# One sine of one column ahead of ScalarE's first work, in a retention, mixer and MLP kernel

## The chip, the cores and the metric

The kernel runs on one core of one Trainium2 chip. The metric is the device time of one execution in microseconds (us); of several executions the median counts.

## The reference

Three layers follow one another, in float32, for 2 batches of 768 tokens with 8 heads of 64 channels (512 channels):

```python
# retention: per head, decaying state
state = gamma * state + k_t (x) v_t ;  y_t = scale * q_t @ state
# mixer with phases
theta = x @ w_theta
zr, zi = x * cos(theta), x * sin(theta)
u = x + (w_tok_r over tokens of zr) + (w_tok_i over tokens of zi)
x = u + relu(u @ w_ch)
# token MLP, then channel MLP
u = x + (relu(x^T @ w_tok1) @ w_tok2)^T
out = u + relu(u @ w_ch1) @ w_ch2
```

ScalarE computes the cosines and sines; everything else that it does is copying, `Abs` and `Relu`.

## The kernel before, in words

Each engine has its own hand-written program (the functions under `block.sync`, `gpsimd`, `scalar`, `vector`, `tensor`), and semaphores order them against one another. A matmul of float32 quality is made of three in the `F32R` type: every operand is split into a high part (a copy in `F32R`) and a low part (the rest), and `three` (L619 to L624) multiplies high with high, high with low and low with high.

The first stage takes the tokens in 12 chunks `g` of 128 (6 for each batch). For a chunk:

- SyncE loads `qkv_in` (`load_chunk`, L241 to L246), three buffers; a weight piece (`load_piece`, L248 to L251, 512 KB, three buffers `stage`) goes between chunks. Both wait on the queue for the work that frees their buffer; piece `i` from the fourth on waits for the low part of piece `i - 3`.
- PE computes the scores (L639), VectorE multiplies them with the decay mask `causal` (`prob`, L473), PE forms the outputs (L669, L679) and the chunk's key-value product (L653). GpSimd multiplies keys with their decay (`k_dec`, L291) and the old state with its decay (`carried`, L300), and VectorE makes the new `state` (L483, L486). VectorE then writes the chunk's result into `res` (L492).
- ScalarE copies that result into `x_hi` (`x_high`, L359), VectorE makes `x_lo` (L497), and PE computes theta: 12 matmuls at L622 with the two pieces of `w_theta` in `w_sq`. Of each weight piece, ScalarE makes the high part (`piece_high`, L352) and VectorE the low part (`piece_low`, L466 or L468). The two pieces of `w_theta` are split in chunk 0, behind that chunk's `x_hi` and `x_lo`.
- theta is folded into half a turn (L367 on ScalarE, L506 and L509 on VectorE); `waves` (L370 to L377) takes `Abs`, a sine for the cosine (with a bias from the constants) and a sine; VectorE multiplies both with the transposed chunk (L515, L518).

In the order written out for VectorE, the mask of chunk `g + 1` (`weigh`) stands ahead of `x_low(g)`. PE's order is at L725 on: the scores of the next chunk come behind the outputs, and theta of a chunk one round later.

From 95 us on PE runs the token mixing, the channel product, the token MLP and the channel MLP, with high parts from ScalarE and low parts from VectorE or GpSimd.

The constants are one array `cst`: ScalarE issues the transfer of its first 277 columns as its first instruction (L388), and SyncE that of the rest. `idle` is a tile of zeros that VectorE writes first of all (L533); PE multiplies it with itself twice while the first chunk is under way. The build puts `ACT_TABLE_LOAD` instructions, which no line of the kernel asks for, into ScalarE's program, each with the line of the activation behind it. In the program before there are two: one ahead of the first copy, and one ahead of the first sine.

ScalarE's program around the change, up to the loop:

Of the kernel before, what the change touches and what calls it, by code (L numbers as in the profile page):

```python
# [7 lines left out]
ACT = mybir.ActivationFunctionType  # L8

P = 128  # L10
# [63 lines left out]
def retention_mixer_mlp(nc, qkv, weights, consts, out):  # L74
    with ExitStack() as ctx:
        def sb(name, shape, dt=F32, within=ctx):
            return within.enter_context(nc.sbuf_tensor(name, shape, dt))

        def sem(name):
            return ctx.enter_context(nc.semaphore(name))  # L80

        cst = sb("cst", [P, N_CONST])
        causal = sb("causal", [P, 2, 4 * P])
        stage = sb("stage", [P, NSTAGE, PIECE])

# [23 lines left out]
        with ExitStack() as warm:  # L109
            idle = sb("idle", [P, DM], within=warm)  # L110
# [72 lines left out]
        idle_ready = sem("idle_ready")  # L183
# [165 lines left out]
        def _(act):  # L349
# [36 lines left out]
                act.activation(u[:, b, 0, k, :], res[:, b, k, :], ACT.Copy).then_inc(ut_hi, 1)  # L386

            act.dma_start(cst[:, 0:C_OUT], consts[:, 0:C_OUT]).then_inc(const_in, 16)  # L388
            act.wait_ge(const_in, 16)
            for g in range(NG + 2):  # L390
                if g < NG:
# [520 lines left out]
```

## Time and profile before

| | |
|---|---|
| median of 3 runs | 461.89 us (461.87 to 463.2) |
| profiled execution, own time | 461.14 us |
| its span, first to last instruction | 459.1 us |
| busy: PE, DVE, POOL, ACT | 449.8, 160.1, 123.3, 104.4 us |

The profile is of one execution, and all times in it count from the start of its span; the 2.0 us between span and time lie outside it. Engines: PE is TensorE, DVE VectorE, ACT ScalarE, POOL GpSimd, SP SyncE. A name such as L622 is a line of the kernel before. "Idle before" is the time in which an engine had nothing to run ahead of an instruction, with the instruction or transfer that ended it.

### The profile page before, as it was taken

The page shows a single profiled execution, that of the slowest core. Times are in us where ns is not written, and L with a number is a line of the kernel's source. Part 1 is how long each engine was busy: PE and PEld are TensorE (multiplying, and loading weights), DVE is VectorE, ACT ScalarE, POOL GpSimd, SP SyncE. Part 2 cuts the span into 40 slices and gives each one's busy share as a digit, 9 for nine tenths or more (in the row PEclk, how much of TensorE's full clock was granted, in tenths as well). Part 3 has the DMA queues.
Part 4 walks back from the last instruction along what each step waited for, and adds up shares of the span by engine and source line. Part 5 has one row for each costly group of instructions (what it writes and reads, how often), then busy time and mean ns, then how long its engine had stood idle before and what let it go on. Part 6 is the DMA issues. An engine that isn't in the chain of part 4 may idle for free.

```text
span 459.1 us, 6208 instructions
## 1 busy us (share of the span) xinstructions
PE 449.8 (98%) x2748; PEld 394.5 (86%) x2748; DVE 160.1 (35%) x227; ACT 104.4 (23%) x157; POOL 123.3 (27%) x80
## 2 busy tenths in 40 slices
PE   7899999999999999999999999999999999999996
PEld 4677877999999999999989988888888888888885
DVE  3789999743211220225335411111311112111112
ACT  0365555632022120002123311111111111111110
POOL 1422320326063141499934880000000000000000
PEclk9999999999999999999999999999999999999999
DMA  8955570042000000044420000000200000200002
GB/s 307 415 216 206 226 275 1 0 129 101 1 0 1 1 0 1 1 140 165 156 91 1 0 1 0 0 1 0 93 0 0 1 0 15 78 0 1 0 0 93
DMA packets 8458, 31.21 MB, mean 68 GB/s; under 512 B 880, under 2 KB 2032, under 8 KB 7024
## 3 DMA queue, kind: packets, MB, share of 16 engines
q1 hardware_dynamic: 8288, 30.67, 18.1%
q8 instruction: 22, 0.36, 0.3%
q10 hardware_dynamic: 144, 0.14, 0.2%
q14 instruction: 4, 0.03, 0.0%
HBM read 27.67 MB, written 3.15 MB: 67 GB/s over the span
## 4 chain that ended last, share of the span: by engine, by line
PE 95%; DVE 2%; DMA 1%; ACT 1%; issue 0%; DVEq 0%; ACTq 0%
PE ps L622 85%; PE ps L679 2%; PE ps L639 2%; PE ps L693 2%; PE ps L776 1%; DMA cst<-consts 1%; PE ps L653 1%; PE ps L669 1%; DVE res L616 1%; DVE prob L473 1%; ACT L359 0%; DVE causal L535 0%; DVE w_sq L468 0%; ACT w_sq L352 0%; DVE z_split L523 0%
## 5 line engine op out<-in xcount | busy, mean ns | idle before, releaser
L622 PE MATMUL ps<-u,w_a 128*128 128x512 f32 x432 | 103.3, 390 | 0.0
L622 PEld LDWEIGHTS ps<-u,w_a 128*128 128x128 f32 x432 | 81.1, 188 | 16.7
L610 DVE SCALAR_TENSOR_TENSOR w_sq<-ps,w_sq 128x512 fp32r<-128x512 f32 x36 | 24.9, 692 | 156.7 <-ACT w_sq L447 156.7
L622 PE MATMUL ps<-w_a,z_split 128*128 128x384 f32 x384 | 68.5, 336 | 0.2 <-DVE z_split L523 0.2
L622 PEld LDWEIGHTS ps<-w_a,z_split 128*128 128x128 f32 x384 | 66.6, 188 | 0.6 <-issue 0.5
L447 ACT ACTIVATE w_sq<-ps 128x512 fp32r<-128x512 f32 x36 | 21.5, 599 | 168.1 <-PE ps L622 168.1
L622 PE MATMUL ps<-w_sq,z_split 128*128 128x512 f32 x216 | 51.9, 389 | 0.0
L622 PE MATMUL ps<-w_sq,w_b 128*128 128x512 f32 x216 | 51.4, 390 | 0.0
L622 PEld LDWEIGHTS ps<-w_sq,z_split 128*128 128x128 f32 x216 | 40.6, 188 | 8.4
L622 PEld LDWEIGHTS ps<-w_sq,w_b 128*128 128x128 f32 x216 | 40.6, 188 | 8.4
L622 PE MATMUL ps<-u,w_sq 128*128 128x384 f32 x192 | 35.1, 338 | 0.0
L622 PE MATMUL ps<-w_b,z_split 128*128 128x384 f32 x192 | 34.4, 335 | 0.0
L622 PEld LDWEIGHTS ps<-w_b,z_split 128*128 128x128 f32 x192 | 33.4, 188 | 0.0
L622 PEld LDWEIGHTS ps<-u,w_sq 128*128 128x128 f32 x192 | 33.2, 188 | 0.0
L622 PE MATMUL ps<-w_sq,x_hi 128*128 128x512 f32 x96 | 30.7, 401 | 1.8 <-DVE w_sq L468 1.8
L530 DVE TENSOR_TENSOR res<-ps,res 128x384 f32<-128x384 f32 x16 | 8.2, 553 | 64.6 <-PE ps L622 64.6
L306 POOL TENSOR_TENSOR z_split<-z,z_split 128x768 fp32r<-128x768 f32 x8 | 15.7, 1959 | 45.1 <-ACT z_split L381 45.1
L291 POOL TENSOR_TENSOR k_dec<-qkv_in,cst 128x512 f32<-128x512 f32 x10 | 13.7, 1373 | 38.8 <-DMA qkv_in<-qkv 38.8
L381 ACT ACTIVATE z_split<-z 128x768 fp32r<-128x768 f32 x16 | 12.6, 838 | 44.2 <-PE ps L622 44.2
L311 POOL TENSOR_TENSOR u<-res,u 128x768 fp32r<-128x768 f32 x8 | 15.4, 1936 | 24.2 <-ACT u L386 24.2
L622 PEld LDWEIGHTS ps<-w_sq,x_hi 128*128 128x128 f32 x96 | 17.2, 189 | 5.0 <-issue 2.0
L622 PE MATMUL ps<-w_sq,x_lo 128*128 128x512 f32 x48 | 18.8, 392 | 0.0
(67 smaller groups left out, 463.7 us busy)
## 6 DMA issues: line engine op xcount, KB each, us to landing
stage<-weights SPq DMA_DIRECT2D x28, 512.0 KB, 3.3
qkv_in<-qkv SPq DMA_DIRECT2D x11, 1024.0 KB, 5.8
cols_out<-res SPq DMA_DIRECT2D x12, 256.0 KB, 2.3
qkv_in<-qkv SPq DMA_DIRECT2D x2, 512.0 KB, 5.1
cst<-consts SPq DMA_DIRECT2D x1, 256.0 KB, 5.7
cst<-consts ACTq DMA_DIRECT2D x1, 138.5 KB, 4.8
```

Source lines behind the costliest of these rows:

```text
L291: pool.tensor_tensor(heads(k_dec[:, n % 2, :]), heads(qkv_in[:, g % NQ, 2 * DM:3 * DM]), key_decay, ALU.mult).then_inc(key_ready, 1)
L306: pool.tensor_tensor(z_split[:, n % 2, 1, 0, :], z_blk[:, n // NK, 0, n % NK, :], f32(z_split[:, n % 2, 0, 0, :]), ALU.subtract).then_inc( ...
L311: pool.tensor_tensor(u[:, b, 1, k, :], res[:, b, k, :], f32(u[:, b, 0, k, :]), ALU.subtract).then_inc(ut_lo, 1)
L381: act.activation(z_split[:, n % 2, 0, a, :], z_blk[:, n // NK, a, n % NK, :], ACT.Copy).then_inc(z_hi, 1)
L447: act.activation(h2[:, f % 2, 0, :], bank(BK_H2 + f % 4), ACT.Relu).then_inc(h2_hi, 1)
L473: dve.tensor_tensor(prob[:, :, :], ps[:, BK_SCORE:BK_SCORE + 2, :], causal[:, :, :], ALU.mult).then_inc(prob_ready, 1)
L530: dve.tensor_tensor(part, ps[:, BK_MIX + 2 * (n % 2) + half, 0:HS], part, ALU.add).then_inc(y_kept, 1)
L610: dve.scalar_tensor_tensor(out=h2[:, f % 2, 1, :], in0=bank(BK_H2 + f % 4), scalar=0.0, in1=f32(h2[:, f % 2, 0, :]), op0=ALU.max, op1=ALU. ...
L622: mm = pe.matmul(dst, left(l), right(r), start=first and n == 0, stop=last and n == 2, skip_group_check=True)
L639: mm = pe.matmul(ps[:, BK_SCORE + r, i * P:(i + 1) * P], qkv_in[rows, g % NQ, DM + i * P:DM + (i + 1) * P], qkv_in[rows, g % NQ, i * P:(i ...
L679: mm = pe.matmul(ps[cols, BK_Y + r, i // 2 * P:(i // 2 + 1) * P], qkv_in[:, g % NQ, 3 * DM + h * D:3 * DM + (h + 1) * D], prob[:, r, i * P ...
L693: mm = pe.transpose(ps[:, BK_XROW, k * P:(k + 1) * P], res[:, b, k, c * P:(c + 1) * P], ident)
```

## The change

ScalarE gets two instructions behind its first transfer: it waits for `idle`, and takes the sine of one column of it. The result goes to a new tile `spare` that nothing reads. `spare` stands behind `cst` in memory.

```diff
         cst = sb("cst", [P, N_CONST])
+        spare = sb("spare", [P, 1])
         causal = sb("causal", [P, 2, 4 * P])
...
             act.dma_start(cst[:, 0:C_OUT], consts[:, 0:C_OUT]).then_inc(const_in, 16)
+
+            act.wait_ge(idle_ready, 1)
+            act.activation(spare[:, :], idle[:, 0:1], ACT.Sin)
             act.wait_ge(const_in, 16)
```

In the memory plan of the built program `spare` takes 32 bytes of each partition: `causal` starts at 19712 in place of 19680, and each later tile 32 bytes higher too. `cst` stays.

Where ScalarE's instructions stand, up to the first sine of the kernel, with the semaphores that each waits for (`x_ready` is set by `res` of L492, `piece_in` by a piece's landing). Before:

```order
L388 DMA cst<-consts 128x277
L359 ACT_TABLE_LOAD [waits x_ready]
L359 ACTIVATE x_hi<-res 128x512 [waits const_in]
L352 ACTIVATE w_sq<-stage 128x1024 [waits piece_in0]
L352 ACTIVATE w_sq<-stage 128x1024 [waits piece_in1]
L359 ACTIVATE x_hi<-res 128x512 [waits x_ready]
L367 ACTIVATE fold<-ps 128x512 [waits theta_ready]
L359 ACTIVATE x_hi<-res 128x512 [waits theta_ready,x_ready]
L372 ACTIVATE fold<-turn 128x512 [waits angle_ready]
L374 ACT_TABLE_LOAD
L374 ACTIVATE fold<-fold,cst 128x512 [waits abs_ready]
L376 ACTIVATE turn<-turn 128x512
```

and ScalarE now, up to the same place (lines are 1 higher up to L387, and 4 higher behind the added ones):

```order
L389 DMA cst<-consts 128x277
L392 ACT_TABLE_LOAD
L392 ACTIVATE spare<-idle 128x1 [waits idle_ready]
L360 ACTIVATE x_hi<-res 128x512 [waits x_ready,const_in]
L353 ACTIVATE w_sq<-stage 128x1024 [waits piece_in0]
L353 ACTIVATE w_sq<-stage 128x1024 [waits piece_in1]
L360 ACTIVATE x_hi<-res 128x512 [waits x_ready]
L368 ACTIVATE fold<-ps 128x512 [waits theta_ready]
L360 ACTIVATE x_hi<-res 128x512 [waits theta_ready,x_ready]
L373 ACTIVATE fold<-turn 128x512 [waits angle_ready]
L375 ACTIVATE fold<-fold,cst 128x512 [waits abs_ready]
L377 ACTIVATE turn<-turn 128x512
```

The first table load now stands ahead of the new sine, without a wait, where it stood behind the wait for `x_ready`; the second is gone, and no other takes its place further on. The instructions of the other engines keep their order.

## Rows read from the trace of the kernel before

**Rows 1.** The page, busy time by engine; and the core's span and mean granted clock.

```profile
PE 449.8 (98%) x2748; PEld 394.5 (86%) x2748; DVE 160.1 (35%) x227; ACT 104.4 (23%) x157; POOL 123.3 (27%) x80
...
core 0: 459.1 us, clock 1.000
```

**Rows 2.** Stretches A:B: us, busy by engine with count, granted clock, DMA share, GB/s.

```profile
15.20:18.20 3.00, 2.99 (x14) 2.25 (x14) 1.42 (x3) 0.00 (x0) 2.47 (x2) 1.00 1.01 408
18.20:20.60 2.40, 2.29 (x50) 1.86 (x50) 1.88 (x3) 1.12 (x2) 0.52 (x1) 1.00 1.04 427
```

**Rows 3.** Waits of PE, before 20.6 us and from there on: us in total, times, longest.

```profile
PE ps L622 <- DVE w_sq L468: 1.8, 1, 1.8
...
PE ps L622 <- DVE z_split L523: 0.2, 1, 0.2
```

**Rows 4.** The chain that ended last, 0 to 31 us: start us, us, what.

```profile
10.25 0.61 DVE res L492
...
10.93 1.28 ACT L359
...
15.21 2.96 PE ps L622 x12
...
21.68 1.09 PE ps L639 x16
```

**Rows 5.** Timeline of ACT: start us, us, instruction, count, idle time before it.

```profile
0.74 0.39 ACTq L388 DMA_DIRECT2D cst<-consts  x1
...
12.22 0.63 ACT L359 ACTIVATE x_hi<-res 128x512 fp32r<-128x512 f32 x1
12.76 1.99 ACT L352 ACTIVATE w_sq<-stage 128x1024 fp32r<-128x1024 f32 x2
...
24.87 1.28 ACT L374 ACT_TABLE_LOAD   x1
...
26.79 0.61 ACT L376 ACTIVATE turn<-turn 128x512 f32<-128x512 f32 x1
...
31.64 0.63 ACT L359 ACTIVATE x_hi<-res 128x512 fp32r<-128x512 f32 x1 [2.80 <-DVE res L492]
```

**Rows 6.** Timeline of DVE: the same columns.

```profile
0.91 0.48 DVE L533 MEMSET idle<- 128x512 f32 x1 [0.91 <-PEq L905]
5.61 1.23 DVE L535 TENSOR_TENSOR causal<-cst 128x1024 f32<-128x1024 f32 x1 [4.21 <-DMA cst<-consts]
...
11.08 1.22 DVE L473 TENSOR_TENSOR prob<-ps,causal 128x1024 f32<-128x1024 f32 x1 [0.23 <-PE ps L639]
12.89 0.69 DVE L497 TENSOR_TENSOR x_lo<-res,x_hi 128x512 fp32r<-128x512 f32 x1 [0.58 <-ACT x_hi L359]
13.84 2.36 DVE L468 SCALAR_TENSOR_TENSOR w_sq<-stage,w_sq 128x1024 fp32r<-128x1024 f32 x2 [0.25 <-ACT w_sq L352]
...
18.11 0.68 DVE L492 TENSOR_TENSOR res<-ps,cst 128x512 f32<-128x512 f32 x1
19.31 1.22 DVE L473 TENSOR_TENSOR prob<-ps,causal 128x1024 f32<-128x1024 f32 x1 [0.52 <-PE ps L639]
20.45 1.22 DVE L497 TENSOR_TENSOR x_lo<-res,x_hi 128x512 fp32r<-128x512 f32 x1
```

**Rows 7.** SP's issues of weight pieces; then KB each, us from issue to landing.

```profile
2.78 1.24 SPq L251 DMA_DIRECT2D stage<-weights  x2
...
15.09 0.33 SPq L251 DMA_DIRECT2D stage<-weights  x1
...
stage<-weights SPq DMA_DIRECT2D x1, 512.0 KB, 8.3
...
stage<-weights SPq DMA_DIRECT2D x1, 512.0 KB, 8.9
```

**Rows 8.** Timeline of POOL: start us, us, instruction, count, idle time before it.

```profile
14.96 2.14 POOL L291 TENSOR_TENSOR k_dec<-qkv_in,cst 128x512 f32<-128x512 f32 x1 [4.02 <-DMA qkv_in<-qkv]
...
20.08 1.04 POOL L291 TENSOR_TENSOR k_dec<-qkv_in,cst 128x512 f32<-128x512 f32 x1 [2.41 <-DMA qkv_in<-qkv]
```

## The prediction

> **What bounds the kernel now.** The page comes first. TensorE (PE) is busy for 449.8 of 459.1 us, ScalarE (ACT) for 104.4 of them, and the granted clock is 1.000 over the whole span, the 2.4 GHz level [rows 1]. So time can only be won where PE stands still. The waits of PE say where that is: from 20.6 us to the end it waits once, for 0.2 us [rows 3], and in the first 20 us its longest wait inside the program's chain is 1.8 us, ahead of the first theta matmul, for VectorE's (DVE's) `w_sq` of L468 [rows 3]. So what ScalarE does after 20.6 us, the twelve chunks' cosines and sines among it, holds PE nowhere.
>
> The chain of waits [rows 4] tells what stands behind the 1.8 us. DVE finishes chunk 0's output (`res` L492) at 10.86; then ScalarE's table load takes 1.28 (10.93 to 12.21), and PE starts theta at 15.21. Between the two stand ScalarE's `x_hi` (12.22, 0.63) and two high parts of `w_sq` from 12.76 [rows 5], and DVE's low part, which starts at 13.84 [rows 6]. The first of the two loads is thus a link of the chain that sets the end. There is a second load, at 24.87 ahead of the first sine [rows 5]. Nothing ran on ScalarE between its DMA issue (done at 1.13) and 10.93, and the load sat behind the semaphore of `x_hi`, so it could not use that time.
>
> **The change, part by part.**
>
> *The load at 10.93 goes to the front.* It costs 1.28 there [rows 4]. Its new place is after ScalarE's DMA issue, from 1.13 on; the sine behind it also waits for `idle`, a memset that ends at 0.91 + 0.48 = 1.39 [rows 6]. No row shows a sine of one column. Above, the 512-column one takes 0.61 [rows 5]; below, nothing. Either way load and sine are over by 1.39 + 1.28 + 0.61 = 3.3 us, over 7 us ahead of ScalarE's first work. Cost on the path: 0; the cover is ScalarE's idle time, and without it the cost would be up to 1.9.
>
> *What of the 1.28 comes through.* `x_hi` starts at 10.93, not 12.22, and ends at 11.56. But DVE is not free: its `prob` of chunk 1 runs from 11.08 to 12.30 [rows 6]. Before, DVE then idled 0.58 for `x_hi`; now `x_lo` starts behind `prob`. So 0.58 of 1.29 comes through, not all. `x_lo` takes 0.69 and ends near 12.99. Two of ScalarE's `w_sq` take 1.99, so the first now runs from 11.47 to about 12.5 and is ready by then, so DVE's second idle stretch, 0.25, goes too. Sum of the two: 0.83. (Where DVE rows follow each other at once, the next starts up to 0.1 before the recorded end of the last (19.31 + 1.22 = 20.53 against 20.45 [rows 6]), so two such places where there were waits add 0 to 0.17.) I take 0.9 of the 0.83 to 1.0: `w_sq` at 12.94, theta at 14.31.
>
> *Do the weights come in time?* Piece 0 is issued at 2.78 and lands 8.3 later, at 11.1; the new need is 11.47. Piece 1, the second of the two issues that take 1.24 together, goes out at 3.4 to 3.5 and takes 8.9: 12.3 to 12.4, against a new need of about 12.4 [rows 7]. The first is covered by 0.4, the second by nothing; but PE wants piece 1 only six matmuls after theta's start (1.4 us), and DVE reaches it after its first low part, at 14.1, so half a microsecond of lateness is free.
>
> *Does 0.9 survive until PE's unbroken run?* Chunk 2 lands just before 14.96, where GpSimd (POOL) stops waiting for it [rows 8], and its request is not touched. POOL then makes `k_dec`, which took 2.14 here and 1.04 for the next chunk, while DVE worked on `w_sq` until 16.20 (13.84 + 2.36). After it stand POOL's `carried`, DVE's `state` and `res`, the last from 18.11 to 18.79, ahead of `prob` at 19.31 [rows 6]. The new `prob` wants to start at 18.41. It can if `k_dec` is shorter. Its 1.10 excess lies where DVE's `w_sq` ran beside it (1.24 us from 14.96); that now ends 0.9 earlier and leaves 0.3 of overlap, so `k_dec` ends near 16.3 and `res` near 18.0: 0.9 survives. If `k_dec` keeps its 2.14, `res` holds `prob` at about 18.8, and 0.5 is left. I take the first, since the row's excess and the overlap are the same size. The Trainium skill (GPSIMD Engine Reference, Specifications) says the same kind of thing, that GpSimd's memory interfaces are shared with VectorE and contend with DVE instructions that have two SBUF inputs; the trace agrees for this row (2.14 against 1.04), and by a view without contention 0.5 would stand in place of 0.9.
>
> *SyncE's queue.* Piece 3's issue waits for the first low part (15.09 [rows 7]) and chunk 4's stands behind it; both leave 0.9 earlier and share the transfers with chunk 3, which lands just before 20.08 [rows 8]. PE's scores wanted that chunk at 21.68 [rows 4] and want it at 20.8 now: 0.7 is left. Nothing here adds a term.
>
> *The load at 24.87 goes away.* 1.28 us of ScalarE, and DVE's products with the cosine come earlier by it. PE waits for neither [rows 3]. What hides it is PE's own queue; were that cover gone, it would be worth its 1.28. Term: 0. `x_hi` copies in 0.63 under the sine's table (31.64) as under the first (12.22) [rows 5], so keeping one table costs nothing.
>
> *The memory.* `spare` takes 32 bytes, so every tile from `causal` on lies 32 bytes higher. No row shows such a shift. Bounds come from the rate of the transfers in the first 20 us, which is 408 GB/s in one stretch and 427 in the next [rows 2]: a change of that spread (4.5%) on the constants' way from 0.74 to about 5.6 is 0.2 us either way. I take 0.
>
> **Sum.** Span 459.1 - 0.9 = 458.2; time of the profiled execution 461.14 - 0.9 = 460.2. The median of the runs shown, 461.89, is 0.75 above that execution, so the prediction for a median is 461.0.
>
> **Rivals.**
> 1. *POOL keeps its pace:* 0.5 comes through, 460.6 by the profile, 461.4 by the median. For it: that the overlap is the cause is read from one row; against it, how well the two sizes match. Chance 0.17.
> 2. *The load gets in the way of the constants (slower).* DVE's first real work waits 4.21 us for ScalarE's own transfer, issued at 0.74 [rows 6]. If the load and the sine hold that transfer's processing by the load's length, 1.28, `causal`, `prob`, PE's outputs and `res` all move by up to 1.28 and `x_hi` is back at 12.2. `prob` of chunk 1 then ends at 13.58, `x_lo` at 14.2, the low part at 15.4, theta starts at 15.55: 0.34 slower than before, 461.5 by the profile, 462.2 by the median. It decides from a delay of about 0.94. Against it: the issue stands ahead of the load, and its 0.39 us are over before it starts. Chance 0.06.
> 3. *The 32 bytes matter for the transfers.* By the bound above 0.2 more or less: 460.8 or 461.2 by the median. Chance 0.08. The Trainium skill (DMA: Bandwidth & Descriptors, How a descriptor splits into AXI transactions) says a descriptor that doesn't start on 256 bytes costs one more transaction. In the built program the tiles behind `cst` start 224 bytes past a multiple of 256, and now on one; by that page rows of 4096 bytes would need 16, not 17, and an estimate from that page is 6% off the first landing, some 0.3 us. No row here shows an aligned tile.
> 4. *The 32 bytes matter for PE's reads.* PE has 2748 matmuls [rows 1]; half a nanosecond each is 1.4 us, and a gain is as possible as a loss. Nothing in the profile speaks for it, and no row excludes it. Time by the median: 459.6 or less, or 462.4 or more. Chance 0.07.
> 5. *The switch costs more than its row.* The Trainium skill (ScalarE: Activation LUTs, What ACT_TABLE_LOAD costs) adds a drain of about 1.38 us to the load, 2.66 in all; by it an estimate would be 458.9 for the profiled execution. The trace differs: `res` ends at 10.86, the load starts at 10.93 [rows 4] and `x_hi` starts 1.29 after that, so at most 0.07 is hidden there. And whatever came on top would be met by DVE's `prob`, which holds `x_lo` at 12.3. As a mechanism here: another 0.07, 460.9. Chance 0.02.
> 6. *No change:* the program still loads at `x_hi`. The built order shows one load and no second. 461.9, chance 0.02.
>
> **How the numbers follow.** The forecast keeps 0.58. A measurement of this kernel can tell about 0.3%, or 1.4 us, from no change. The forecast and rivals 1, 2, 3, 5 and 6 lie within that. Only rival 4 reaches beyond, about evenly; with runs that scatter (one of three was 463.2) I give faster 0.05, same 0.90, slower 0.05. The range runs from the forecast with rival 3's gain and the profiled execution's offset from the median, 461.0 - 0.2 - 0.75, rounded to 460.1, to rival 2 at 462.2.
>
> **What would show it.** Right: one table load, at about 1.2 to 2.7; the first `x_hi` at 10.9; DVE's `x_lo` behind `prob` with no idle time; theta's first matmul at 14.3 and PE's wait ahead of it near 0.9 in place of 1.75; POOL's third `k_dec` at 1.3 to 1.4; `prob` of chunk 2 at 18.4; all of PE's later rows 0.9 earlier; a span of 458.2. Wrong: `causal` later than 5.6 (rival 2); `k_dec` still at 2.1 with `prob` at 18.8 (rival 1); other mean durations for the 512-column matmuls (rival 4); or a new PE wait for chunk 3 near 20.7.

## The result

The median of 6 executions of the changed kernel is 459.31 us (459.07 to 459.72), against 461.88 us of the kernel before (460.64 to 463.2 in 6). The ratio is 0.9943, with a 95% interval of 0.9926 to 0.996: 2.57 us, or 0.57%, faster. That is outside the stated range (460.1 to 462.2) and beyond the 1.4 us that bounded "the same". In the four sets of the experiments below, the kernel before has 92 executions with a median of 462.3; the changed kernel has 12, these six and six of a later set, with a median of 459.4.

The profiled execution took 459.27 us with a span of 457.2, so 1.9 less than the 459.1 before. The page's busy row and the core's row, changed kernel:

```profile
PE 449.5 (98%) x2748; PEld 394.3 (86%) x2748; DVE 159.5 (35%) x227; ACT 103.4 (23%) x157; POOL 121.7 (27%) x80
...
core 0: 457.2 us, clock 1.000
```

PE has 0.3 us less work and 1.9 us less span [rows 1]; the other 1.6 was idle time. Lines of the changed kernel are higher by 1 up to L387 and by 4 behind: L626 is L622 of before. Waits of PE, before 20 us and in all; then the chain that ended last (start us, us, what):

```profile
PE ps L626 <- DVE w_sq L472: 0.7, 1, 0.7
...
10.66 0.60 DVE res L496
11.25 1.22 DVE prob L477
...
14.35 2.96 PE ps L626 x12
...
20.83 1.09 PE ps L643 x16
```

The wait ahead of theta fell from 1.8 to 0.7 [rows 3], and ScalarE is no longer in the chain: it goes from `res` over DVE's `prob` to theta at 14.35 (15.21 in [rows 4]). ScalarE's, VectorE's and GpSimd's timelines, with the columns of [rows 5]:

```profile
1.16 1.28 ACT L392 ACT_TABLE_LOAD   x1 [1.16 <-PEq L909]
2.45 0.20 ACT L392 ACTIVATE spare<-idle 128x1 f32<-128x1 f32 x1
11.35 0.63 ACT L360 ACTIVATE x_hi<-res 128x512 fp32r<-128x512 f32 x1 [8.70 <-DVE res L496]
11.89 1.99 ACT L353 ACTIVATE w_sq<-stage 128x1024 fp32r<-128x1024 f32 x2
...
12.39 0.68 DVE L501 TENSOR_TENSOR x_lo<-res,x_hi 128x512 fp32r<-128x512 f32 x1
12.99 2.35 DVE L472 SCALAR_TENSOR_TENSOR w_sq<-stage,w_sq 128x1024 fp32r<-128x1024 f32 x2
...
18.46 1.23 DVE L477 TENSOR_TENSOR prob<-ps,causal 128x1024 f32<-128x1024 f32 x1 [0.52 <-PE ps L643]
...
14.96 1.29 POOL L292 TENSOR_TENSOR k_dec<-qkv_in,cst 128x512 f32<-128x512 f32 x1 [3.91 <-DMA qkv_in<-qkv]
```

The one load runs from 1.16 and the sine takes 0.20. `x_lo` follows `prob` with no idle time (0.58 in [rows 6]), and `w_sq` follows `x_lo` with none (0.25 before). `k_dec` took 1.29 in place of 2.14 [rows 8], and `prob` of chunk 2 starts at 18.46 (19.31). Up to 31 us all this is the forecast: PE is 0.85 to 0.88 ahead (20.83 against 21.68). But at the start of PE's unbroken run (the token mixing and all behind it, in which PE never stands still) the lead is 1.43, and the span ends 1.9 earlier. The kernel before, chain from 46 us on and VectorE's timeline:

```profile
46.14 1.03 PE ps L679 x16
...
48.26 0.06 issue
48.32 0.63 PE ps L693 x4
...
55.02 0.08 issue
55.10 0.63 PE ps L693 x4
...
47.49 0.68 DVE L518 TENSOR_TENSOR z<-ps,turn 128x512 f32<-128x512 f32 x1
```

The changed kernel, the same two views:

```profile
45.29 0.88 PE ps L683 x16
...
47.26 0.59 PE ps L697 x4
...
45.49 0.68 DVE L522 TENSOR_TENSOR z<-ps,turn 128x512 f32<-128x512 f32 x1
```

Before, PE's transposes of chunk 4 (L693; the first chunk is 0) start at 48.32, 0.15 after VectorE's product L518 of chunk 3 ends (47.49 + 0.68 = 48.17), for which they have to wait. The wait is 0.06 to 0.08 and stands in the chain as "issue", four times (48.26, 55.02 and two more, for chunks 4 to 7), with the transposes 0.04 longer each time. VectorE's lateness shows once more just ahead of them: the outputs of chunk 6 (L679), which need VectorE's `prob`, take 1.03 from 46.14, and 0.88 in the changed kernel (45.29). Together this is the 0.57 by which the lead grows: 0.15, and four times about 0.1. In the changed kernel VectorE is done at 46.17 and PE comes at 47.26, 1.1 later. The second load had used up that margin. The last part is in rows of the whole chain, before and then after:

```profile
95.94 110.51 PE ps L622 x636
...
453.50 2.73 DVE res L616 x4
```

```profile
94.51 110.50 PE ps L626 x636
...
451.96 2.73 DVE res L620 x4
```

From the unbroken run's start to the last additions PE needs 357.56 before and 357.45 after, and from the end of the additions to the end of the span it is 459.1 - 456.23 = 2.87 before and 457.2 - 454.69 = 2.51 after. Neither has anything to do with a table, as e1 and g1 to g3 will show.

### The profile page after: what moved, and what is told of

Same layout as the page of the kernel before. It is cut to its first block, busy times and chain, and to the rows that moved or that the text cites. A ratio compares the mean times of both kernels' runs of the same rounds, so it can differ in the third digit from the quotient of the medians.

```text
span 457.2 us, 6208 instructions
## 1 busy us (share of the span) xinstructions
PE 449.5 (98%) x2748; PEld 394.3 (86%) x2748; DVE 159.5 (35%) x227; ACT 103.4 (23%) x157; POOL 121.7 (27%) x80
## 4 chain that ended last, share of the span: by engine, by line
PE 96%; DVE 2%; DMA 1%; issue 0%; DVEq 0%
PE ps L626 86%; PE ps L643 3%; PE ps L683 2%; PE ps L697 1%; PE ps L780 1%; DMA qkv_in<-qkv 1%; PE ps L657 1%; PE ps L673 1%; DVE prob L477 1%; DVE res L620 1%; DVE w_sq L472 0%; DVE z_split L527 0%; DVE z L519 0%; DVE x_lo L501 0%; DVE z L522 0%
## 5 line engine op out<-in xcount | busy, mean ns | idle before, releaser
L626 PE MATMUL ps<-u,w_a 128*128 128x512 f32 x432 | 103.3, 389 | 0.0
L626 PEld LDWEIGHTS ps<-u,w_a 128*128 128x128 f32 x432 | 81.1, 188 | 16.8
L626 PE MATMUL ps<-w_a,z_split 128*128 128x384 f32 x384 | 68.5, 335 | 0.2 <-DVE z_split L527 0.2
L626 PEld LDWEIGHTS ps<-w_a,z_split 128*128 128x128 f32 x384 | 66.6, 188 | 0.6 <-issue 0.5
L626 PE MATMUL ps<-w_sq,z_split 128*128 128x512 f32 x216 | 51.9, 389 | 0.0
L626 PE MATMUL ps<-w_sq,w_b 128*128 128x512 f32 x216 | 51.4, 389 | 0.0
L626 PEld LDWEIGHTS ps<-w_sq,w_b 128*128 128x128 f32 x216 | 40.5, 188 | 8.4
L626 PEld LDWEIGHTS ps<-w_sq,z_split 128*128 128x128 f32 x216 | 40.5, 188 | 8.4
L626 PE MATMUL ps<-u,w_sq 128*128 128x384 f32 x192 | 35.0, 337 | 0.0
L626 PE MATMUL ps<-w_b,z_split 128*128 128x384 f32 x192 | 34.4, 334 | 0.0
L626 PEld LDWEIGHTS ps<-w_b,z_split 128*128 128x128 f32 x192 | 33.4, 188 | 0.0
L626 PEld LDWEIGHTS ps<-u,w_sq 128*128 128x128 f32 x192 | 33.1, 188 | 0.0
L626 PE MATMUL ps<-w_sq,x_hi 128*128 128x512 f32 x96 | 30.7, 401 | 0.7 <-DVE w_sq L472 0.7
L307 POOL TENSOR_TENSOR z_split<-z,z_split 128x768 fp32r<-128x768 f32 x8 | 15.7, 1958 | 45.8 <-ACT z_split L382 45.8
L292 POOL TENSOR_TENSOR k_dec<-qkv_in,cst 128x512 f32<-128x512 f32 x10 | 12.5, 1253 | 41.8 <-DMA qkv_in<-qkv 41.8
L626 PEld LDWEIGHTS ps<-w_sq,x_hi 128*128 128x128 f32 x96 | 17.2, 188 | 4.0 <-issue 0.9
L626 PE MATMUL ps<-w_sq,x_lo 128*128 128x512 f32 x48 | 18.8, 392 | 0.0
```

Of the source, the lines that this page charges most:

```text
L292: pool.tensor_tensor(heads(k_dec[:, n % 2, :]), heads(qkv_in[:, g % NQ, 2 * DM:3 * DM]), key_decay, ALU.mult).then_inc(key_ready, 1)
L307: pool.tensor_tensor(z_split[:, n % 2, 1, 0, :], z_blk[:, n // NK, 0, n % NK, :], f32(z_split[:, n % 2, 0, 0, :]), ALU.subtract).then_inc( ...
L626: mm = pe.matmul(dst, left(l), right(r), start=first and n == 0, stop=last and n == 2, skip_group_check=True)
```

## The experiments

They ran in four sets, each set on one chip beside the kernel before. Theories: **A**, each load costs, the first on the chain, the second through VectorE's margin; **B**, the 32 bytes cost or gain; **C**, PE's early gaps let its clock fall in part of the executions; **D**, those falls come regardless; **E**, without margin VectorE's chance delays reach PE.

### Tile alone, sine alone, copy, sine behind the wait (e1 to e4)

e1 is the kernel before with the tile only:

```diff
         cst = sb("cst", [P, N_CONST])
+        spare = sb("spare", [P, 1])
```

> The tile alone, no sine: every later tile 32 bytes higher, both table loads where they were. Theory A (both loads count: the first 0.86 us on the chain, the second 0.54 us through the slack of VectorE's phase work; the tile nothing): time as before, 461.9, ratio 1.000; theta(0) near 15.2; PE's transposes of chunks 5 to 8 (L693 before) still start some 0.06 us late, near 48.3, 55.1, 61.9, 68.7. Theory B (the 32 bytes count for what the first load does not explain: 0.54 between 42 and 69 us, 0.1 in the channel product, 0.36 after the last addition): 1.0 us faster, about 460.9, ratio 0.998, with the last output landing 2.5 us after the last addition instead of 2.9.

e2 has the sine and no moved tile (the constants' tile has room for a column):

```diff
-        cst = sb("cst", [P, N_CONST])
+        cst = sb("cst", [P, N_CONST + 1])
...
+            act.wait_ge(idle_ready, 1)
+            act.activation(cst[:, N_CONST:N_CONST + 1], idle[:, 0:1], ACT.Sin)
```

> The sine at the front, its result into a padding column of the constants' tile, so no tile moves. Theory A: as the changed kernel, about 459.3, ratio 0.9943; theta(0) near 14.35, token mixing's unbroken run from 94.5. Theory B: only the first load's 0.86 comes through, about 461.0, ratio 0.998; theta(0) near 14.35, unbroken run from 95.1, last output landing 2.9 us after the last addition.

e3 is e2 with a copy, so that the first load moves and the second stays:

```diff
-            act.activation(cst[:, N_CONST:N_CONST + 1], idle[:, 0:1], ACT.Sin)
+            act.activation(cst[:, N_CONST:N_CONST + 1], idle[:, 0:1], ACT.Copy)
```

> As e2, but a copy of one column in place of the sine: the first load goes to the front, the second stays at the first sine (24.9 before, about 24 now). Theory A: theta(0) near 14.35, but PE's transposes late again from chunk 5 on, unbroken run from 95.1 in place of 94.5: about 0.55 slower than e2. The forecast's own view (second load free): same as e2, unbroken run from 94.5.

e4 has one load too, but behind the wait for the first chunk, in `x_high`:

```diff
                 act.wait_ge(x_ready, g + 1)
+                if g == 0:
+                    act.wait_ge(idle_ready, 1)
+                    act.activation(cst[:, N_CONST:N_CONST + 1], idle[:, 0:1], ACT.Sin)
```

> The sine of one column right behind the wait for the first chunk's result: one load only, left on the chain at 10.9, 0.2 us of sine added to the chain, the second load gone; no tile moves. Theory A: theta(0) at 15.2 to 15.4, transposes not late, unbroken run from 95.4 to 95.6 (before: 95.94), so 0.3 to 0.5 faster than before: about 461.4. The forecast's own view (second load free): 0 to 0.2 slower than before, unbroken run from 95.9 to 96.1.

Measured, beside a median of 462.21 for before (35 executions): e1 461.60 (ratio 0.9989, 0.997 to 1.0009), e2 459.71 (0.995, 0.9928 to 0.9972), e3 460.26 (0.9956, 0.9937 to 0.9975), e4 462.91 (1.0004, 0.9982 to 1.0026). So the sine does nearly all, the tile alone is not told from nothing, and with the second load left in, 0.55 of it is gone again (0.65 if the executions with a low clock, of which more below, are left out: 459.60 and 460.25). The chain of e3 shows how:

```profile
45.18 0.18 issue
45.36 1.09 PE ps L682 x16
...
47.54 0.06 issue
47.60 0.63 PE ps L696 x4
...
67.88 0.07 issue
67.95 0.63 PE ps L696 x4
```

PE's transposes (L696 here) are late from chunk 4 to chunk 7, as in the kernel before, though theta(0) starts at 14.21: its way from there to the unbroken run is 81.01 us, against 80.16 in the changed kernel. Of these 0.85, the outputs of chunk 6 (0.18 + 1.09 against 0.88) are 0.39 and the four late transposes the rest. That is A. e4 has A's trace as well (no late transposes), but its median is 1.5 us above the 461.4 that A gave it. Its trace, and that of e1, shows why; stretches with the columns of [rows 2], e1:

```profile
13.60:15.30 1.70, 0.00 (x0) 0.00 (x0) 1.45 (x3) 1.31 (x2) 0.54 (x1) 1.00 1.03 419
...
16.60:19.50 2.90, 2.90 (x7) 1.84 (x6) 1.63 (x3) 0.63 (x1) 1.08 (x1) 0.50 1.02 396
```

PE stood still for 1.99 us up to 15.37, went on, and from 16.6 to 19.5 its granted clock was 0.50, the 1.2 GHz level; theta took 4.76 us there, not 2.96. The page of the kernel before has no such stretch, and its mean clock is 1.000 [rows 1]; but each execution of the four sets comes with its mean clock. It is under 0.9975 in 10 of 12 of e4, 8 of 12 of e1 and 21 of 35 of before; in e2 in 4 of 12 and in e3 in 1 of 12. That gave theory C. In e2 the four with a low clock took 461.2 to 461.4, the others 459.4 to 459.8.

### Gaps filled, a delay in the load's place (e5 to e8)

> The changed kernel once more, beside the others of this set. Theory C (what the traces at full clock do not explain of the 2.57 us comes from executions whose granted clock falls for some 3.5 us in the first 20 us: after PE's gap of 1.75 us ahead of theta(0) it does so in more than half of the executions, after the gap of 0.73 rarely): at most 3 of 12 executions with a mean granted clock under 0.9975, against more than half of those of before; median 459.2 to 459.8. Theory D (the falls come and go without regard to that gap): as large a share here as before.

e6 is the kernel before with work for PE ahead of theta(0); the added matmuls multiply zeros:

```diff
                 if g == 1:
+                    keep_warm(2, 384)
                     theta(0)
```

> The kernel before, both table loads in place, with two matmuls of zeros, 384 columns each, ahead of theta(0): some 1.3 us of the 1.75 us gap filled, nothing else moved. Theory C: the low-clock executions become rare (at most a third), and the median falls from about 462.2 to the full-clock value of before, 461.0 to 461.6. Theory D: share and median as before, 462.2.

e7 is the changed kernel with both early gaps filled:

```diff
             for g in range(NG):
...
+                if g == 0:
+                    keep_warm(1, 448)
                 outputs(g)
...
                 if g == 1:
+                    keep_warm(1, 256)
                     theta(0)
```

> The changed kernel with one matmul of zeros (256 columns) ahead of theta(0) and one (448 columns) ahead of the first outputs, where PE waits 1.4 us for VectorE's first mask product: both gaps nearly closed. Theory C: no execution with a mean granted clock under 0.9975; median as the full-clock executions of the changed kernel, 459.3, so equal to e5 or some tenths faster. Theory D: the same share as e5. If a filling matmul outlasts its gap, theta or the outputs start some tenths late and the time is that much longer.

e8 is the changed kernel with two copies in the second load's place, in `waves`:

```diff
                 act.activation(fold[:, g % 2, :], turn[:, g % 2, :], ACT.Abs).then_inc(abs_ready, 1)
+                if g == 0:
+                    for i in range(2):
+                        act.activation(z[:, 1, 1, :, NC - 1 - i, :], blocks(idle[:, :]), ACT.Copy)
```

> The changed kernel, one table load at the front, with two copies of 512 columns (some 1.15 us) on ScalarE where the second load used to be, behind the first chunk's absolute value. Theory A (the second load costs by its time on ScalarE, which uses up the slack between VectorE's phase work and PE's transposes): PE's transposes late again from chunk 5 or 6 on, the unbroken run of token mixing 0.3 to 0.5 us later than the changed kernel's 94.5, time 0.3 to 0.6 above e5. Rival (the table switch itself slows what follows, not its time): as e5.

Measured, with 462.35 for before (17 executions, 12 of them under 0.9975): e5 460.06, 3 of 6 under 0.9975; e6 462.54, 3 of 12; e7 459.35 (ratio 0.9921, 0.99 to 0.9943), 0 of 6; e8 459.39, 1 of 6. e5 taken alone favours D: half of six, where the changed kernel's first six had none. Its trace shows another gap at work:

```profile
6.40:7.90 1.50, 0.02 (x2) 0.00 (x0) 1.46 (x2) 0.00 (x0) 1.04 (x1) 1.00 1.07 451
...
9.00:11.50 2.50, 2.50 (x32) 2.38 (x30) 0.70 (x2) 0.00 (x0) 1.04 (x1) 0.50 1.04 428
```

There PE idled 1.5 us for the first mask product, ahead of the first outputs, and the clock was at 0.50 from 9.0 to 11.5. The change doesn't touch that gap. e6 brings the share of low executions from 12 of 17 to 3 of 12 by filling the other one, and e7, with both filled, has none. e6's median missed C's 461.0 to 461.6 all the same: its full-clock executions run up to 462.94.

e8's ScalarE rows, and its chain at chunk 5:

```profile
23.90 1.14 ACT L376 ACTIVATE z<-idle 128x512 f32<-128x512 f32 x2
...
47.03 0.06 issue
47.09 0.63 PE ps L700 x4
```

1.14 us of copies make the transposes late (L700), for three chunks in place of four, and the way from theta(0) to the unbroken run is 80.48: 0.32 more than without. So in the trace ScalarE's time at that place is enough to make them late, without any table switch. The copies are 0.14 shorter than the load and bring less than half of e3's 0.85: the outputs of chunk 6 are hardly late (0.91). And the time does not show them: at full clock 459.32, as the changed kernel, where A gave 0.3 to 0.6 more. That no part of the second load's price is an after-effect of the switch is thus likely and not shown.

### Full clock, two by two (f1 to f4)

f1 is before with both gaps filled (448 columns, and twice 384); f2 is e4, f3 is e3 and f4 is the changed kernel, filled alike (f2 twice 448, f3 and f4 once 256 ahead of theta).

> The kernel before with both table loads, and both early gaps of PE filled with matmuls of zeros (448 columns ahead of the first outputs, twice 384 ahead of theta(0)), so that the clock should stay up and only the loads' own cost is left. Theory C: at most 1 of 12 executions with a mean granted clock under 0.9975. Theory E (with the second load in place VectorE's phase work has no slack, so that whatever stretches it, such as a product on POOL that starts beside the clamp at L509, reaches PE): the full-clock executions spread over more than 1 us, from about 461.0 to 462.5, median 461.2 to 461.9. Rival (the spread of before comes from the clock alone): all within 0.5 us, near 461.0.

> As f1, but with the one-column sine behind the wait for the first chunk's result, so that the first load stays on the chain (with 0.2 us of sine) and the second is gone. Theories A and E: transposes not late; PE's unbroken run at theta(0)'s start plus 80.2 us; median 460.2 to 460.8, 0.8 to 1.4 below f1, and all executions within 0.8 us of one another. The forecast's own view (second load free): 0 to 0.2 us slower than f1.

> As the changed kernel with its gaps filled, but a one-column copy in place of the sine: first load at the front, second still at the first sine. Theories A and E: transposes late from chunk 5 on, theta(0)'s start plus 80.8 to 81.0; median 460.0 to 460.6, 0.8 below f1 and 0.7 to 1.1 above f4, with some executions 0.7 us above the rest. The forecast's own view: as f4.

> The changed kernel with both gaps filled, once more (as e7). Theories A, C and E: no execution under 0.9975 of mean granted clock, median 459.3, all within 0.8 us of one another. Theory D (clock falls regardless of the gaps): a quarter or more of the executions under 0.9975.

| | executions | median | lowest, highest | clock under 0.9975 |
|---|---|---|---|---|
| f1, both loads in place | 12 | 461.71 | 460.37, 462.75 | 0 |
| f2, first on the chain, second gone | 12 | 461.17 | 460.50, 461.90 | 0 |
| f3, first moved, second in place | 12 | 460.24 | 459.95, 461.72 | 0 |
| e7, f4 and g4, neither (with tile) | 17 | 459.27 | 458.84, 459.75 | 0 |

C and E hold for f1: no low clock, and yet a spread of 2.4 us. f2 missed its 460.2 to 460.8, with 1.4 between its executions where 0.8 was expected, and f3 came 1.47 below f1 where 0.8 was expected. f1's trace has two reasons (the profiled executions of f1 and f2 were the slowest of their twelve). The first is in its chain:

```profile
14.41 3.22 DVE w_sq L468 x2
...
17.68 1.66 PE ps L622 x6
```

VectorE's two low parts of `w_theta` took 3.22 in place of 2.36 [rows 6], for the second took 2.07 in place of 1.22, beside POOL's `k_dec` and `carried`. PE then waited 0.3 for the second piece, and theta(0) took 3.54 in all and not 2.96. Seven of the 18 traces have this (e1, e2, e4, e5, e6, f1 and f2): the seven in which the low parts start at 13.96 or later. In the other eleven they start at 13.84 at the latest. `k_dec` begins at 14.6 to 15.7 in all 18. (In the profiled execution before, it was `k_dec` that took longer, 2.14, and the low part did not.) So the first load on the chain can cost 0.6 more than its place in the chain says. At full clock it did so in three of four traces with that load there (e6, f1, f2, not in the profiled execution before) and in none of ten without. It is also what f2's trace lost: its way is 80.77, 0.6 more than the 80.2 that A gave it.

The second is in GpSimd's and VectorE's rows:

```profile
50.54 1.05 POOL L291 TENSOR_TENSOR k_dec<-qkv_in,cst 128x512 f32<-128x512 f32 x1 [5.95 <-DMA qkv_in<-qkv]
...
50.76 1.10 DVE L509 TENSOR_SCALAR turn<-turn 128x512 f32<-128x512 f32 x1
```

A chunk landed at 50.5, POOL's `k_dec` began, and DVE's clamp L509 beside it took 1.10, where it takes 0.43 to 0.56 for nearly every other chunk of this stage up to 81 us. In f1 the way from theta(0) to the unbroken run is 81.91, 1.2 more than the 80.73 before, and in e6, whose clamp took 1.31, it is 81.98; 0.6 of it is the late second piece, so the clamp cost 0.6 to 0.7. f4's trace has the same accident (1.25, at 48.1) and pays 80.54 against 80.19 in e7, 0.35. So the margin takes part of it, not all, against E's plain form.

### The tile (g1 to g4)

g1 is f4 with the result in the constants' tile, as in e2; g2 and g3 are f4 with `spare` of 16 and 24 columns; g4 is f4.

> As f4 (sine at the front, both gaps filled), but with the sine's result in a padding column of the constants' tile, so that no tile moves. In the ten traces so far the last output lands 2.5 us after the last addition with the 32-byte tile and 2.8 to 2.9 without, and PE's run from token mixing to the last sum takes 357.45 with it and 357.56 without. Theory B, narrowed to these two places (the tile is worth 0.45 us): 357.56 and 2.8 to 2.9 here, median 459.5 to 459.7, 0.45 above g4. Rival (a chance of the traces): as g4.

> As f4, with the tile for the sine's result 64 bytes wide: later tiles start 32 bytes past a multiple of 256 (before: 224 past; in f4: on a multiple). If the gain comes from tiles on a multiple of 256 or 64 bytes: 2.8 to 2.9 from the last addition to the end of the span and 357.56 for PE's run, median 459.5 to 459.7. If any shift does: as g4.

> As f4, with the tile 96 bytes wide: later tiles start 64 bytes past a multiple of 256. If a multiple of 64 is what counts: 2.5 and 357.45, median 459.0 to 459.3. If it takes a multiple of 256: 2.8 to 2.9 and 357.56, median 459.5 to 459.7.

> The kernel of f4 once more, beside g1 to g3 on the same chip: 2.5 and 357.45, median 459.0 to 459.4, no execution under 0.9975 of mean granted clock.

| later tiles start past a multiple of 256 by | traces | PE's run | last addition to end | time, median |
|---|---|---|---|---|
| 224 bytes (as before) | 9 | 357.53 to 357.56 | 2.79 to 2.87 | g1 459.44 |
| 0 (as changed) | 7 | 357.45 to 357.46 | 2.48 to 2.55 | g4 459.30 |
| 32 | 1 | 357.45 | 2.79 | g2 459.79 |
| 64 | 1 | 357.45 | 2.89 | g3 459.54 |

The transfers' rows of the last four outputs (KB each, median us from issue to landing), before and then after:

```profile
cols_out<-res SPq DMA_DIRECT2D x4, 256.0 KB, 2.3
```

```profile
cols_out<-res SPq DMA_DIRECT2D x4, 256.0 KB, 2.1
```

The output transfer is 0.2 us quicker in the seven traces in which the later tiles start on a multiple of 256 bytes (2.1), and neither of the two other shifts does that (2.3, as before). The Trainium skill (DMA: Bandwidth & Descriptors, How a descriptor splits into AXI transactions) would have it so: a descriptor that starts off such a multiple needs one transaction more. By an estimate from that page the 2048-byte rows of the output would take 9 and not 8. The trace's 2.3 against 2.1 agrees with that in direction, and a tenth is near the eighth. PE's 0.1 us comes with any of the three shifts, and its cause stays open. In the times the tile's share is smaller than in the traces: 0.14 between g1 and g4, whose executions overlap, where the traces say 0.45.

g2 and g3 also hold what the medians hide: five of their 12 executions took 460.0 to 460.51 at full clock, against none above 459.75 of the 17 with the 32-byte tile. g2's profiled execution, the slowest of its six, had two long clamps (0.94 at 42.0, 1.02 at 48.9), late transposes, and a way of 81.05. So two such clamps cost 0.9 with one load too. On the same chip g1 and g4 had no such execution in 11; whether the two shifts make the accident more frequent, no run here tells.

## Why the prediction was wrong

*What held.* Where the first load goes and that it is hidden there (1.16 to 2.44, sine 0.20), that VectorE's `prob` lets only part of it through, both idle stretches of VectorE gone, the weights in time, `k_dec` shorter (1.29; rival 1 is out), chunk 3 in time, the constants not held (`causal` at 5.73 against 5.61, by a landing at 5.7; rival 2 is out), no drain beside the load (rival 5; the trace has the load at 1.28 and the sine at once behind it). That theta(0) came 0.86 earlier, against the 0.9 of the forecast, is luck in part: in the changed kernel's profiled execution `res` of chunk 0 started 0.40 later (10.57 against 10.17), and counted from `res` the gain was 1.26.

*The step that failed: "The load at 24.87 goes away. [...] Term: 0."* At full clock it is 0.54 alone (f1 to f2, with the sine's time against it) and 0.80 once the first is moved (f3 to g1, which ran on two chips; on f3's own chip it is 1.17 to f4, with the tile in it). In the traces it is 0.57 (the way of 80.73 against 80.16) to 0.85 (e3). I read "PE waits for neither" from the list of waits, which leaves out pieces of 0.06 to 0.08; they stood in the chain as "issue", four times ahead of the same line. VectorE's and ScalarE's round for a chunk takes 6.77 us there (`res` at 50.95 and 57.72) and PE's 6.68 where it doesn't wait (47.26 to 53.94 in the changed kernel), so PE gains on it by 0.1 a chunk. VectorE's rounds shrink to 5.3 (`res` at 64.51 and 69.82) once the last of the six weight pieces of this stretch is split, from 61.84 on, and 1.28 us of load decide whether PE catches up before that. That the cover was thin would have been seen by setting L518's end (48.17) beside L693's start (48.32).

*The first load: mis-sized.* 0.9 forecast; 1.47 between the medians of f1 and f3. In the traces with the load in place theta(0) starts 5.03 to 5.04 after the start of chunk 0's `res` (5.12 with the sine of e4 and f2), and in those without, always 3.10 or 3.11 after chunk 1's `prob`. So the gain is 1.94 less the distance from `res` to `prob`. That is 0.91 in the profiled execution before, since chunk 1 landed late and `prob` waited 0.23, and 0.67 when it doesn't, as in the changed kernel: 1.03 or 1.27. Part of what I took for a term of the kernel was one of the execution. The remaining 0.2 of the 1.47 stays open. A candidate is theta(0)'s 0.6, which the first load on the chain brought in three of four traces at full clock: I had priced the load by its place in the chain alone. The traces show that it comes, not how often.

*The memory.* 0.45 in the traces (0.34 at the last output, 0.11 in PE's run), 0.1 to 0.2 in the times, where I had taken 0 and looked for it at the first transfers. The 0.11 is rival 4's kind of effect, at less than a tenth of the 1.4 that it was given.

*The clock* was in no rival. A stretch at 1.2 GHz is in 57 of the 92 executions of before in the four sets, in 3 of 12 of the changed kernel, and in 0 of 71 of the kernels with both gaps filled. For the six executions behind 461.88 it isn't recorded, but for the profiled one, which has none. The 35 of before at full clock have a median of 461.64, so the medians carry 0.7 of it in the four sets (462.3 for all) and perhaps 0.2 in the 461.88; the means are 462.6 and, for f1, 461.6. That the gap of 0.73 in place of 1.75 lowers the share is shown by e6 and by the comparison of e1 and e4 with e2 and e3 (18 of 24 against 5 of 24).

At full clock the way from f1 to the 17 executions with neither load is 2.44 of the measured 2.57, and the runs between split it into 1.47 for the first load, 0.80 for the second and 0.17 for the tile. The sum is no proof of the parts: they are differences of one row of medians, over three chips. On f1's own chip they are 1.47 and, for second load and tile together, 1.17. The rest is of the size that the clock and the chips leave open.

**A steadier version** is the changed kernel with both gaps filled (e7, f4, g4): 17 executions with a median of 459.27 and a highest of 459.75, against 12 of the changed kernel with 459.4 and 460.94. It beats the kernel before; the medians don't tell it from the changed kernel. The executions above 460.5 (3 of 12) didn't come in the 17, which is few to call them gone.

## What to carry to other kernels

Run one tiny activation of the set that the whole kernel can use while the first data is under way: the load takes its 1.28 us there, and not behind the semaphore of the first real work. Before a stall on a second engine is costed at nothing, set the end of what PE needs from it beside PE's start, chunk by chunk: a repeated "issue" of less than 0.1 us ahead of the same line is a wait, and a loop that is 0.1 us a round slower than PE turns a delay at 25 us into lost time at 46 to 69. And size a term on more than one execution where a transfer's landing stands next to it: a landing also decides what runs beside what, and here work that began 0.1 us later met another engine's product and cost PE 0.6.

## What was not expected of the hardware

- PE's granted clock fell to 0.50 (1.2 GHz) for some 3.4 us, 0.1 to 1.2 us after PE had resumed from 1.5 or 2.0 us of standing still within the first 20 us, in some executions of one kernel and not in others. With matmuls of zeros in both gaps no execution of 71 had a mean clock under 0.998.
- VectorE's clamp of 128x512 took 0.43 where no GpSimd product was running at its start, even when one started 0.03 us after it (g3, 48.42 and 48.45). Where one was running, the clamp ended 0.27 to 0.30 after it, in all 97 such cases of the 18 traces, and so took what was left of the product and 0.3 more: 0.56 as a rule, 0.90 to 1.31 beside a `k_dec` that had started up to 0.42 before, and 1.78 beside POOL's `z_split` (85.51 in the kernel before).
- VectorE's low part of 128x1024 took 2.07 beside `k_dec` in f1, and 1.22 without.
- The last output's landing was 2.1 us from tiles on a multiple of 256 bytes, and 2.3 from tiles 32, 64 or 224 bytes past one.
